# Inputs laid out by the host, and attention's loop rearranged, in an attention and two-mixer kernel

## The reference, cut to what matters

```
scores = q k^T / 8, kept where |i-j| < 16;  plus q . (max of k over each block of 32) / 8 + log 32
a      = softmax over both;   x = a [v ; mean of v over each block of 32]     # 2 batches, 8 heads, 768 x 64
h      = relu(x w_in); u, v = halves of h;  v_n = (v - mean) / sqrt(var + 1e-6)
g      = u * (w_spatial v_n + b)
h2     = relu(g (w_out w_in2));  c = convolution of h2 over 3 tokens
out    = (h2 * sigmoid(c)) w_out2                                            # 2 x 768 x 512
```

## Time and profile before

| | us |
|---|---|
| median of 3 runs (lowest, highest) | 375.81 (374.57, 377.02) |
| the profiled execution | 374.59 |
| its span | 372.6 |
| PE busy | 350.8 (94%) |
| DVE, ACT, POOL busy | 223.2, 138.2, 73.0 |

### The profile page before, as it was taken

One profiled execution on the slowest core, in us unless ns is written; L12 is line 12 of the kernel. 1 busy time (PEld: TensorE's weight loads), 2 busy tenths in 40 slices (PEclk: granted clock), 3 DMA queues, 4 the chain that ended last, 5 costly groups with the idle time before them and its releaser, 6 DMA issues.

```text
span 372.6 us, 6760 instructions
## 1 busy us (share of the span) xinstructions
PE 350.8 (94%) x2613; PEld 312.4 (84%) x2613; DVE 223.2 (60%) x572; ACT 138.2 (37%) x398; POOL 73.0 (20%) x87
## 2 busy tenths in 40 slices
PE   6598686989999999999999999999999999999996
PEld 6377565868889889999999988999999988889984
DVE  2759688596258367247644462368775557756662
ACT  3848577484255336341111122421222123122111
POOL 4314456364000000069100094000000000000000
PEclk9969899699999999999999999999999999999999
DMA  9999789864000201365100000000000003100004
GB/s 180 202 186 193 180 193 190 166 157 103 5 0 3 84 1 24 111 201 174 56 2 0 2 0 0 2 0 2 1 0 2 0 0 115 55 2 1 0 2 169
DMA packets 51604, 25.75 MB, mean 69 GB/s; under 512 B 44252, under 2 KB 46580, under 8 KB 51572
## 3 DMA queue, kind: packets, MB, share of 16 engines
q1 hardware_dynamic: 51572, 25.32, 29.1%
HBM read 20.98 MB, written 3.15 MB: 65 GB/s over the span
## 4 chain that ended last, share of the span: by engine, by line
PE 83%; DVE 5%; SPq 4%; issue 3%; ACT 2%; DMA 1%; ACTq 0%; DVEq 0%
PE bank L868 24%; PE bank L870 24%; PE bank L869 24%; PE bank L853 3%; ACT P L487 2%; PE bank L805 2%; PE bank L841 2%; DVE pT L628 2%; DVE SM L648 1%; PE bank L813 1%; SPq L277 1%; PE bank L909 1%; SPq L270 1%; PE bank L831 1%; DMA vw<-vs_s 1%
## 5 line engine op out<-in xcount | busy, mean ns | idle before, releaser
L870 PE MATMUL bank<-g_h,W_l 128*128 128x384 f32 x128 | 43.0, 336 | 0.0
L869 PE MATMUL bank<-g_l,W_h 128*128 128x384 f32 x128 | 42.9, 335 | 0.0
L868 PE MATMUL bank<-g_h,W_h 128*128 128x384 f32 x128 | 42.8, 334 | 0.0
L487 ACT ACTIVATE P<-SM,nmax 128x120 f32<-128x120 f32 x96 | 36.7, 384 | 12.6 <-DVE nmax L648 12.0
L870 PE MATMUL bank<-wo_h,hg_l 128*128 128x512 f32 x96 | 38.0, 396 | 0.0
L869 PE MATMUL bank<-wo_l,hg_h 128*128 128x512 f32 x96 | 38.0, 396 | 0.0
L868 PE MATMUL bank<-wo_h,hg_h 128*128 128x512 f32 x96 | 37.9, 395 | 0.0
L414 POOL TENSOR_TENSOR P<-P,rinv 128x480 f32<-128x480 f32 x24 | 23.7, 987 | 45.9 <-DVE rinv L635 45.9
L868 PE MATMUL bank<-wsT_h,vn_h 128*128 128x384 f32 x96 | 32.2, 335 | 0.0
L869 PE MATMUL bank<-wsT_l,vn_h 128*128 128x384 f32 x96 | 32.1, 334 | 0.0
L870 PE MATMUL bank<-wsT_h,vn_l 128*128 128x384 f32 x96 | 32.1, 334 | 0.0
(11 more groups left out here) (111 smaller groups left out, 803.5 us busy)
## 6 DMA issues: line engine op xcount, KB each, us to landing
stage<-in_moe_w_in SPq DMA_DIRECT2D x8, 512.0 KB, 4.3
vw<-in_v SPq DMA_DIRECT2D x16, 240.0 KB, 4.8
kn<-in_k SPq DMA_DIRECT2D x16, 192.0 KB, 3.6
qn<-in_q SPq DMA_DIRECT2D x16, 192.0 KB, 4.1
stage<-in_moe_w_out SPq DMA_DIRECT2D x6, 512.0 KB, 3.6
out<-obuf SPq DMA_DIRECT2D x12, 256.0 KB, 2.0
stage<-in_moe_w_spatial SPq DMA_DIRECT2D x6, 384.0 KB, 3.9
vw<-vs_s SPq DMA_DIRECT2D x32, 36.0 KB
```

The lines of the kernel that those rows point to most:

```text
L487: a.activation(P[:, i % NP_, j, :], SM[:, i % 2, j, :], ACT.Exp, bias=nmax[:, c:c + 1], scale=-1.0, accum_out=rsum[:, c:c + 1]).then_inc(e ...
L868: t_.matmul(dst, lhs[0](c), rhs[0](c), start=first, stop=False)
L869: t_.matmul(dst, lhs[0](c), rhs[1](c), start=False, stop=False)
L870: ins = t_.matmul(dst, lhs[1](c), rhs[0](c), start=False, stop=last)
```

## The change

The host hands over q, k and v turned to features by tokens, k with its borders repeated for each tile (`kw`, 1440 columns of 4 B a partition and pair), v in windows (`vw`), and v once more by features (`vT`); `w_spatial` and `w_out` come transposed and `conv_w` in its final form. All turning on PE apart from P's is gone, with the copies that followed it and the four `vs_s` DMAs of a pair. DVE takes the block sums of `vT` (`value_sums`), one matmul with the identity turns them, ACT copies them, and POOL spreads them and the key maxima. One bank each holds turned P and outputs. ACT copies two of three `pT`. DVE's order in a slot is now: pT (one group of three), x_l of group i-4, reciprocals of group i-1, key maxima or value sums, masks of group i. No unit of the later stages runs in attention's last slots; W units go ahead of the s units; the wo2 splits lie beside the s units of batch 1. There are three weight slices in flight where there were four, POOL splits `w_in` and `w_out` in 18 parts during attention, and POOL splits v_n.

```diff
+        fills_at = {i: [] for i in range(SLOTS)}
         for p in range(NP):
...
-            units_of[GP * p] = [("k", p + 1, 0), ("k", p + 1, 1)] if more else []
...
-            units_of[GP * p + 1] = (vs if p > 0 else []) + ([("q", p + 1, 0)] if more else [])
-            units_of[GP * p + 2] = ([("q", p + 1, 1)] if more else []) + (vs if p == 0 else [])
...
+            fills_at[max(1, GP * p)].append(("vs", p))
+        b0 = [("v", 0, m) for m in range(SC6)] + [("u", 0, f, n) for f in range(FC) for n in range(2)]
+        seq = [u for i in range(SLOTS) for u in fills_at[i]]
+        ATT = len(seq)
+        seq += b0
+        seq += [("v", 1, m) for m in range(SC6)]
+        seq += [("u", 1, f, n) for f in range(FC) for n in range(2)]
+        seq += [("W", f, n) for n in range(2) for f in range(FC)]
+        for b in range(B):
+            seq += [("s", b, f, n) for f in range(FC) for n in range(2)]
+        place = {u: n for n, u in enumerate(seq)}
...
+        items = [("wi", c) for c in range(KC)] + [("wo", c) for c in range(KC // 2)] + [("w2", c) for c in range(KC)]
+        items += [("ws", c) for c in range(SC6)] + [("wo2", c) for c in range(GC // 2)]
...
+                if p >= 2:
+                    sp.wait_ge(qk_done, GP * (p - 1))
+                sp.dma_start(kw[:, p % 2, :, :], kw_in[p]).then_inc(k_in[p % 2], 16)
...
+            load_k(0)
+            load_vT(0)
             load_k(1)
             load_q(1)
+            load_item(0)
             load_v(0)
+            load_vT(1)
+            load_item(1)
             load_v(1)
...
+            for p in range(2, NP):
+                load_vT(p)
+                load_k(p)
+                load_q(p)
+                load_v(p)
...
+            def spread_keys(p):
+
+                pool.wait_ge(ks_ready, p + 1)
+                g.tensor_copy(kw[:, p % 2, :, KW:KA],
+                              ks[:, p % 2, :].unsqueeze(1).to_broadcast([128, NT, NB])).then_inc(kw_ready, 1)
+
+            def spread_sums(p):
+
+                pool.wait_ge(vsum_ready, p + 1)
+                pool.wait_ge(kw_ready, p + 2 if p == 0 else min(p + 1, NP))
+                if p >= NVB:
+                    pool.wait_ge(pv_done, GP * (p - NVB + 1))
+                if n_hi:
+                    pool.wait_ge(split_hi, n_hi)
+                src = vsum[KW:KA, p % 2, :].unsqueeze(1).to_broadcast([NB, NT, 2 * D])
+                g.tensor_copy(vw[KW:KA, p % NVB, :, :], src).then_inc(vw_ready, 1)
+                pool.wait_ge(vw_ready, p + 1)
+
+            parts = [(x, part) for x in items[:KC + KC // 2] for part in range(3)]
+            spread_keys(0)
+            for i in range(1, NG + 1):
+                n = i - 1
+                pool.wait_ge(rinv_ready, n + 1)
+                pi = P[:, n % NP_, :, :]
+                g.tensor_tensor(out=pi, in0=pi, in1=rinv[:, n * GT:(n + 1) * GT].unsqueeze(2).to_broadcast([128, GT, KA]),
+                                op=ALU.mult).then_inc(norm_done, 1)
+                if i % GP == 2 and i // GP + 1 < NP:
+                    spread_keys(i // GP + 1)
+                p = i // GP if i > 2 else 0
+                if i == 2 or i > 2 and i % GP == 1 and p < NP:
+                    pool.wait_ge(norm_done, i)
+                    spread_sums(p)
+                if i >= 2:
+                    for _ in range((2, 0, 1)[i % GP]):
+                        if parts:
+                            split_part(*parts.pop(0))
...
+            act.dma_start(qT[:, 0, :], qT_in[0]).then_inc(q_in[0], 16)
...
+            for i in range(SLOTS):
+                if i >= 4:
+                    n = i - 4
                     p, r = divmod(n, GP)
                     act.wait_ge(pv_done, n + 1)
-                    c0 = (p // PPB) * S + r * GT * TQ
-                    a.activation(x_h[:, p % PPB, c0:c0 + GT * TQ], OT[n % 2][:, 0:GT * TQ], ACT.Copy).then_inc(xh_ready, 1)
...
+                    c0 = r * GT * TQ
+                    a.activation(x_h[p // PPB][:, p % PPB, c0:c0 + GT * TQ], OT[:, 0:GT * TQ], ACT.Copy).then_inc(xh_ready, 1)
+                if 3 <= i < NG + 3 and (i - 3) % GP > 0:
+                    n = i - 3
+                    act.wait_ge(pt_done, n + 1)
+                    if n >= 2:
+                        act.wait_ge(pv_done, n - 1)
+                    a.activation(pT[:, n % 2, :], PTB[0:KA, :], ACT.Copy).then_inc(pT_act, 1)
...
+            def key_maxima(p):
+                dve.wait_ge(k_in[p % 2], 16 * (p // 2 + 1))
+                if p >= 2:
+                    dve.wait_ge(kw_ready, p - 1)
+                vv.tensor_reduce(out=ks[:, p % 2, :].rearrange("p (t j) -> p t j", j=2),
+                                 in_=kw[:, p % 2, :, WINDOW:WINDOW + TQ].rearrange("p t (j s) -> p t j s", s=BLOCK),
+                                 op=ALU.max, axis=AX.X).then_inc(ks_ready, 1)
+
+            def value_sums(p):
+                dve.wait_ge(vT_at[p % 2], 16 * (p // 2 + 1))
+                if p >= 2:
+                    dve.wait_ge(ring_done, done_count(("vs", p - 2)))
+                vv.tensor_reduce(out=vb[:, p % 2, :], in_=vT[:, p % 2, :].rearrange("p (n s) -> p n s", s=BLOCK),
+                                 op=ALU.add, axis=AX.X).then_inc(vb_ready, 1)
+
...
+            key_maxima(0)
+            for i in range(SLOTS):
+                if 3 <= i < NG + 3 and (i - 3) % GP == 0:
                     n = i - 3
                     dve.wait_ge(pt_done, n + 1)
                     if n >= 2:
                         dve.wait_ge(pv_done, n - 1)
-                    vv.tensor_copy(pT[:, n % 2, :], PTB[n % 2][0:KA, :]).then_inc(pT_ready, 1)
+                    vv.tensor_copy(pT[:, n % 2, :], PTB[0:KA, :]).then_inc(pT_dve, 1)
+                if i >= 4:
+                    n = i - 4
+                    p, r = divmod(n, GP)
+                    b, c0 = p // PPB, r * GT * TQ
+                    dve.wait_ge(xh_ready, n + 1)
+                    vv.tensor_tensor(out=x_l[b][:, p % PPB, c0:c0 + GT * TQ], in0=OT[:, 0:GT * TQ],
+                                     in1=x_h[b][:, p % PPB, c0:c0 + GT * TQ].bitcast(fp32),
+                                     op=ALU.subtract).then_inc(xl_ready, 1)
                 if 1 <= i <= NG:
                     n = i - 1
+                    cols = slice(n * GT, i * GT)
                     dve.wait_ge(exp_done, GT * i)
...
+                    vv.tensor_scalar(rinv[:, cols], rsum[:, cols], 1e-9, None, ALU.add).then_inc(den_ready, 1)
                     dve.wait_ge(den_ready, i)
...
+                    vv.reciprocal(rinv[:, cols], rinv[:, cols]).then_inc(rinv_ready, 1)
+                if i % GP == 1 and i // GP + 1 < NP:
+                    key_maxima(i // GP + 1)
+                if i % GP == 2 and i // GP + 1 < NP:
+                    value_sums(i // GP + 1)
                 if i < NG:
                     dve.wait_ge(qk_done, i + 1)
...
+                    if i >= NP_:
+                        dve.wait_ge(pt_done, i - NP_ + 1)
                     if i == 0:
                         dve.wait_ge(mask_ready, 3)
...
                     for j in range(GT):
                         e, h = divmod(j, 2)
                         t, c = i % GP * 2 + h, i * GT + j
                         kind = FIRST if t == 0 else LATEST if t == NT // 2 - 1 else INNER
...
-                        vv.tensor_tensor_reduce(out=SM[:, i % 2, j, :], in0=SC[e][:, at:at + KA],
-                                                in1=mask[:, kind, :], scale=-1.0, scalar=LARGEST, op0=ALU.add,
+                        vv.tensor_tensor_reduce(out=P[:, i % NP_, j, :], in0=SC[e][:, h * KA:(h + 1) * KA],
+                                                in1=mask[:, kind, :], scale=-SCALE, scalar=LARGEST, op0=ALU.add,
                                                 op1=ALU.min, accum_out=nmax[:, c:c + 1]).then_inc(max_ready, 1)
-                if i >= 5:
...
-                    c0 = (p // PPB) * S + r * GT * TQ
-                    vv.tensor_tensor(out=x_l[:, p % PPB, c0:c0 + GT * TQ], in0=OT[n % 2][:, 0:GT * TQ],
...
+                if i == 0:
+                    value_sums(0)
...
+                if what == "vs":
+                    ins = t_.matmul(bk[KW:KA, 0:2 * D], vb[:, u[1] % 2, :], ident[:, :], start=True, stop=True)
...
+            for i in range(SLOTS):
                 if i < NG:
                     scores(i)
+                if 2 <= i < NG + 2:
+                    transpose_probs(i - 2)
+                for u in fills_at[i]:
+                    dense(u)
+                if 3 <= i < NG + 3:
+                    values(i - 3)
+            for u in seq[ATT:]:
+                dense(u)
...
```

More of the change, by code:

```diff
@@ L91, in attention_mixer_program @@
             [("wi_h", [128, KC, F], f32r), ("wi_l", [128, KC, F], f32r)],
[L92 to L96, removed]
+            [(f"wsT_{x}{c}", [128, S], f32r) for c in range(SC6 - 1) for x in "hl"],
+            [("hbuf", [128, 2, S + 2], fp32), ("cbuf", [128, 2, S], fp32),
```

(40 more changed lines are left out.)

770 lines of the change are left out of this document (276 added, 494 removed).

## The result

The changed kernel takes 379.67 us (median of 4 runs, 379.43 to 380.41) against 375.51 (374.57 to 377.02) for the kernel before on the same chip: ratio 1.011, 95% interval 1.0073 to 1.0148. The profiled execution took 379.43 and its span is 377.6, 5.0 more than before. The page has fewer busy microseconds on PE and more on POOL. The DMA engines are less full during the loads: three slices of the span stand at 9 where five did. From the eleventh slice on neither kernel has more than 6 in one.

A forecast was written before the change was run, and what follows sets the result against it. Attention (no engine full throughout), then PE's column count behind it, were taken to bound the kernel. Terms -1.8 + 3.5 + 4.5 + 3.5 - 6.2 + 0.6 + 1.5 = +5.6 on 374.6 gave 380.2, forecast 380, range 370 to 387.

The forecast's parts named there:

- The start: Ahead of attention's loop: first keys land at 5.3, first exponential at 7.9 instead of 9.68, -1.8 us (-0.8 to -2.4).
- The loop: First to last group's exponential in attention: x_h, x_l, reductions and ACT's copy lengthen slots, 80.9 against 77.4, +3.5 us.
- Rival 2: Attention's loop: x_h and x_l stay off it as before and nothing is held, 363.3 us; chance 0.13.
- The port: Attention's loop: a DVE addition is held until POOL's split ends, 0.8 to 1.0 in five or six rounds, +4.5 us.
- rival 1: Attention's loop: POOL holds nobody and the clock stays up, 374.2 us; chance 0.24.
- The end: Last group's first exponential to first v unit: 7.3 us with nothing filling it, then four u units, 15.7 for 12.2, +3.5.
- PE behind: From the first v unit on: the turning of w_spatial, w_out and conv_w goes from PE, -6.2 us.
- the term of 0.6: Behind the s units: first gate_in now follows s, and the second gate_in waits for its bank, +0.6 us (0 to +2).
- The clock: PE in attention and first units: one fall to half clock near the end, +1.5 us; 5.0 in full.
- Rival 3: PE's clock: half all through attention and into the first units, 383.7 us; chance 0.14.
- Rival 4: Loads in attention: they stay at the old rate, 113 us of loading, over 400 us; no separate chance given.
- k(p) is late for nobody: Key loads in attention: issued when scores of pair p-2 end, read over 6 us later, against some 4 us to land.

The follow-up runs named there:

- the fastest kernel: Changed kernel with x_l behind the masks and two output banks, reductions behind the masks, thinner POOL splits, four v units in attention's end: 358.82 us, ratio 0.9608.

## Why the prediction was right, point by point

**The sum.** +5.6 was forecast, the span grew by 5.0, and the time came out at 379.67 for 380. That closeness is in part luck. The start was taken 2.0 too low and the loop without its hold 0.8 too low; the hold and the clock were taken 2.7 too high, the end and what follows it 0.7.

**The start: wrong.** The failed step is the landing of the first keys. I had inferred 2.1 us of latency from the old keys at 200 GB/s, but then gave the new keys 1.9 us for 0.74 MB, some 390 GB/s, with 5.3 as their landing and -1.8 as the gain. They were read at 6.82, and without SP's later loads at 6.62. At the 200 GB/s of the old keys the same sum gives 0.74 + 2.1 + 3.7 = 6.5 (an estimate from the prediction's own terms). Even the 2.1 is not a measured latency: before, PE went from its first turns of the identity to those of the keys without a stop, so 4.85 is only the latest time at which the keys can have landed. The rest of the step was taken a little low, 2.6 for the 3.05 that it took: the first scores took 1.08 us for 16 instead of 0.65, after PE had stood idle for 3.2 us. With 28 first turns instead of 16 they took 0.64, and from the read of the keys to the first exponential it was 9.64 - 7.03 = 2.61 us. Before, the first turning needed two loads of 0.2 MB each, and now the maxima need 0.74 MB, since the borders come with the keys; that this is why the new layout gives nothing here is my reading, and wasn't tried.

**The loop: right, by its own rows.** Forecast 80.9 without the hold and 85.4 with it; measured 81.7 and 85.0. Rounds are 11.20, where near 11.8 was forecast. A slot with nothing added was put at 3.0 and takes 2.90; one with value sums 3.87 and takes 3.72; one with maxima and ACT's copy 4.12 and takes 4.16 once the hold is gone. The steady steps lie 0.1 to 0.15 under the forecast, and what made up for it were two waits for loads in the first four steps, 0.42 for value sums and 0.98 for keys, which the sum had at nothing. Both pieces were taken out singly and their time went: x_h and x_l (11.2 with the bank, 7.4 without), reductions (11.4). Rival 2, that x_h and x_l stay off the loop, falls: DVE waits for x_h 23 times.

**The port: right in kind, a third too dear.** I had 0.8 to 1.0 in five or six rounds, 4.5. Seven additions were held, to 0.92, 0.64 and five times 0.58, so (0.76 + 0.48 + 5 x 0.42) = 3.3 us above 0.16. In the five, the addition came 3.34 us behind the one before it rather than 3.0, since ACT's copy of the sums stands ahead of x_h in just these slots, and less of the split was left. With one split in a slot the 0.42 went from the step. That also answers rival 1, that POOL holds nobody. By the Trainium skill, SBUF — State Buffer, section Who interferes with whom, of a VectorE instruction in a two-port mode and a GpSimd instruction the one that issues later is blocked until the other is over; the trace agrees, up to 1.23 for 0.17. The reciprocals take 0.18 in every kernel here, also in the seven cases where one starts during a split of POOL, and the reductions take 0.95 at most.

**The end: right.** 7.3 forecast, 7.1 measured, and the four units behind it. But PE was idle for 2.8 of it, not for most. Filling it gave 2.8.

**PE behind: right.** 272 to 273 us forecast, 272.3 measured from the first v unit's start to the last gate_out's end (374.26). The turning of weights is gone. From the first gate_in to the first gate_out it was 12.66 for 12.51, so the term of 0.6 was 0.15.

**The clock: too much.** I took 1.5 for one fall near the end. The granted clock was at half for much of attention (mean 0.77 as recorded, and less by the durations of the scores), more than before, and the loop didn't feel it; in the profiled run the end and the first units ran at full clock. In five other kernels of this study it fell there, and the v units of batch 0 took 17.5 to 17.7 us for 16.4, so the term is real in some programs, at 1.1 to 1.3. The forecast had 1.7 to 3.4 for such a fall, from 3.4 to 6.8 us at half clock: rows 9 show the 6.8, and no row or run shows the 3.4. Rival 3's half clock throughout attention came, but not its price.

**The loads.** Rival 4, the old rate, fell with 318 GB/s and no DMA wait behind pair 2. But "k(p) is late for nobody", on some 4 us to land, was wrong for pair 2 (the median of the eight key loads is 4.4): its keys were read 9.4 us after issue, 0.98 of it as a stop. In the fastest kernel they came 11.0 us after issue, and the stop was 2.66.

## What to carry to other kernels

In this loop, taking work away from PE, which didn't set its pace, bought nothing; what counted was the order of DVE's and ACT's programs, where each instruction between the last exponential and the next mask costs its whole length in every slot. Put what nobody awaits (x_l, block maxima, block sums) behind the instruction that the other engine awaits, and pay with one more bank where the order needs it. A change that removes the work which filled a drain must name what fills it next.

## What the runs showed of the hardware that was not expected

- A tiny VectorE addition (128x4, 0.16 us) took up to 1.23 us beside POOL's splits and up to 0.75 beside its copy of the value sums, on the path of every later slot. A reciprocal of the same 128x4 took 0.18 in all seven cases in which it started during a split.
- The first load of 0.74 MB was read 5.9 us after its issue with nothing of SP's behind it, and 5.8 to 6.7 after it in the ten profiles with ten loads behind it.
- With a mean recorded clock of 0.98 in attention instead of 0.77 the loop's steps were 4.58, 3.72 and 2.90 in both: PE had that much slack. In the second profile of the changed kernel the clock was 0.72, and the steps were the same.
- The recorded clock can miss a fall: in the changed kernel it stands at 1.00 up to 30 us, where 16 scores take 1.08 us, and in its second profile it stands at 0.50 from 10 to 20 us beside the same 1.08. The durations of small matmuls tell the clock there, the record doesn't.
